# Attention in a fused kernel: the shared block as two 64-column couples, reciprocals widened and transposed, and three moves of order

## What is computed

```
scores = scale * matmul(q, k.T)                        # 4 batches x 8 heads, 576 x 64
thresh = max(scores, -1) - tau
scores = where(scores >= thresh, scores, -1e9)
attn   = exp(scores - max(scores)); attn /= sum(attn) + 1e-9
x      = matmul(attn, v)                               # -> 2304 x 512
h      = relu(x @ w_in);  x = (h * h) @ w_out          # 512 -> 2048 -> 512
e      = argmax(x @ w_gate)                            # 8 experts
out    = gate * sigmoid(x @ w_output_gate)[e] * ((x @ w1[e]) @ w2[e])
```

## Time and profile before

| | |
|---|---|
| median of 3 runs | 1035.98 us (1035.89 to 1037.17) |
| the profiled execution | 1037.33 us, of which span 1035.5 |
| TensorE busy | 1004.8 us, 97% of the span |
| VectorE, ScalarE, GpSimd busy | 617.7, 590.7, 414.1 us |
| granted TensorE clock, mean | 0.997 |
| attention | the first 333 us |

### The profile page before, as it was taken

One profiled execution on the slowest core, in us unless ns is written; L12 is line 12 of the kernel. 1 busy time (PEld: TensorE's weight loads), 2 busy tenths in 40 slices (PEclk: granted clock), 3 DMA queues, 4 the chain that ended last, 5 costly groups with the idle time before them and its releaser, 6 DMA issues.

```text
span 1035.5 us, 19649 instructions
## 1 busy us (share of the span) xinstructions
PE 1004.8 (97%) x6923; PEld 835.6 (81%) x6923; DVE 617.7 (60%) x1204; ACT 590.7 (57%) x922; POOL 414.1 (40%) x725
## 2 busy tenths in 40 slices
PE   7999999999998999999999999999999999999996
PEld 5877877877876788888888888889978888888884
DVE  5778787877876433422322242234788777777773
ACT  4777777777776332322322232223548888888883
POOL 4777777777776000000000000000007666666763
PEclk9999999999999999999999999999999999999998
DMA  4222232332210310021002001103579256451110
GB/s 114 76 63 63 75 70 53 72 84 53 70 40 22 93 51 21 1 52 31 1 21 55 7 1 42 40 1 83 183 269 396 105 203 240 153 194 41 33 41 34
DMA packets 85387, 84.07 MB, mean 81 GB/s; under 512 B 49711, under 2 KB 64559, under 8 KB 85298
## 3 DMA queue, kind: packets, MB, share of 16 engines
q1 hardware_dynamic: 81778, 72.41, 23.7%
q0 software_dynamic: 3520, 10.49, 3.0%
HBM read 69.24 MB, written 15.21 MB: 82 GB/s over the span
## 4 chain that ended last, share of the span: by engine, by line
PE 65%; DVE 1%; SPq 0%; issue 0%; DMA 0%; ACT 0%; POOL 0%; ACTq 0%; POOLq 0%
PE y_ps L1163 19%; PE h_ps L1146 19%; PE y_ps L1227 15%; PE row_ps L1227 7%; PE h_ps L1258 2%; PE row_ps L1132 2%; PE y_ps L1217 1%; DMA y_rows<-r_buf 0%; SPq L965 0%; SPq L961 0%; PE h_ps L1132 0%; POOL out_dram L1054 0%; DVE y_row L1697 0%; DVE g_lo L1484 0%; DVE g_buf L1479 0%
## 5 line engine op out<-in xcount | busy, mean ns | idle before, releaser
L1479 DVE TENSOR_TENSOR g_buf<-r_buf 128x512 f32<-128x512 f32 (+1 forms) x80 | 51.1, 639 | 222.0 <-ACT r_buf L1331 221.3
L1331 ACT ACTIVATE r_buf<-h_ps 128x512 f32<-128x512 f32 (+1 forms) x80 | 44.4, 555 | 235.3 <-PE h_ps L1146 231.8
L947 POOL TENSOR_TENSOR w_lo<-w_experts,w_hi 128x2048 fp32r<-128x2048 f32 x20 | 125.1, 6255 | 78.3 <-ACT w_hi L1390 78.2
L1390 ACT ACTIVATE w_hi<-w_experts 128x2048 fp32r (+1 forms) x100 | 150.4, 1564 | 0.5 <-PE row_ps L1227 0.5
L1065 POOL MEMSET ones<- 128x128 bf16 x1 | 0.2, 209 | 357.9 <-DVE x_lo L1465 357.9
L947 DVE TENSOR_TENSOR w_lo<-w_experts,w_hi 128x1024 fp32r<-128x1024 f32 (+1 forms) x80 | 136.9, 1753 | 4.5 <-ACT w_hi L1390 4.2
L476 ACT ACTIVATE e_sb<-s_sb,stats,live 128x576 f32<-128x576 f32 x144 | 124.5, 866 | 20.9 <-POOL stats L262 19.6
L1146 PE MATMUL h_ps<-x_hi,w_in_hi 128*128 128x512 f32 (+1 forms) x320 | 119.9, 375 | 2.3 <-DVE x_lo L1465 2.3
L1163 PE MATMUL y_ps<-g_hi,w_out_hi 128*128 128x512 f32 (+1 forms) x320 | 118.0, 369 | 1.6 <-DVE g_lo L1484 1.6
L1146 PE MATMUL h_ps<-x_hi,w_in_lo 128*128 128x512 f32 (+1 forms) x320 | 117.9, 369 | 0.0
L1146 PE MATMUL h_ps<-x_lo,w_in_hi 128*128 128x512 f32 (+1 forms) x320 | 117.8, 368 | 0.0
(11 more groups left out here) (250 smaller groups left out, 2226.1 us busy)
## 6 DMA issues: line engine op xcount, KB each, us to landing
w_experts<-in_moe_w_dram SPq DMA_DIRECT2D x18, 2048.0 KB, 9.6
y_rows<-y_row SPq DMA_DIRECT2D x36, 128.0 KB, 2.5
k_raw<-in_k_dram SPq DMA_DIRECT2D x32, 128.0 KB, 3.1
q_raw<-in_q_dram SPq DMA_DIRECT2D x32, 128.0 KB, 3.0
w_raw<-in_moe_w_in_dram SPq DMA_DIRECT2D x16, 256.0 KB, 3.1
v_nat<-in_v_dram SPq DMA_DIRECT2D x16, 256.0 KB, 2.7
y_T<-in_moe_w_out_dram SPq DMA_DIRECT2D x16, 256.0 KB, 2.8
y_early<-y_row SPq DMA_DIRECT2D x32, 128.0 KB, 2.4
```

What stands on the lines that cost most here:

```text
L947: alu.tensor_tensor(group_of(w_lo, g)[:, c0:c1], raw_group(buf, g)[:, c0:c1], group_of(w_hi, g)[:, c0:c1].bitcast(F32), ALU.subtract).then ...
L1390: nc.scalar.activation(group_of(w_hi, g)[:, c0:c1], raw_group(buf, g)[:, c0:c1], ACT.Copy).then_inc(hi_done, 1)
L1479: V.tensor_tensor(g_buf[:, 0:cols], r_buf[:, 0:cols], r_buf[:, 0:cols], ALU.mult).then_inc(sq_done, 1)
```

## The change

Five edits, all in attention.

1. The product with `v_mix` is made as two products of 64 columns, one for each half of the array, in place of one of 128.
2. `rinv` grows from nine numbers per partition to nine times 64. The reciprocal reads each sum 64 times and writes it 64 times.
3. `broadcast_rinv` makes four 128 x 128 transposes of `rinv` in place of eight 64-column products with the identity.
4. On TensorE `output_tail` stands ahead of the third transpose set of its step.
5. On VectorE the reciprocal stands ahead of `k_lo`; on GpSimd `add_eps` stands ahead of `cuts`.

```diff
-        rinv = sb("rinv", [P, CHUNKS])
+        rinv = sb("rinv", [P, CHUNKS, D])
...
                     biases(i, c)
-                    cuts(i, c)
                     if c == 0 and i >= 1:
                         add_eps(i - 1)
+                    cuts(i, c)
...
-                pe.matmul(o_ps[:, cols], v_mix[b][:], pt[:, LAST, :], start=False, stop=(c == LAST - 1),
-                          skip_group_check=True).then_inc(pv_done, 1)
+                for par in range(2):
+                    last = pe.matmul(o_ps[D * par:D * (par + 1), cols], v_mix[b][:, D * par:D * (par + 1)], pt[:, LAST, :],
+                                     start=False, stop=(c == LAST - 1), skip_group_check=True)
+                last.then_inc(pv_done, 1)
...
                 for c in range(LAST):
-                    for par in range(2):
-                        last = pe.matmul(m_ps[D * par:D * (par + 1), c * P:(c + 1) * P],
-                                         rinv[:, 2 * c + par:2 * c + par + 1].broadcast_to([P, D]), ident[:],
-                                         start=True, stop=True)
+                    last = pe.transpose(m_ps[:, c * P:(c + 1) * P],
+                                        rinv[:, 2 * c:2 * c + 2, :].rearrange("p h d -> p (h d)"), ident[:])
...
+                if 0 <= used[0] and used[1] == LAST:
+                    output_tail(used[0])
                 if 0 <= made[0] < PAIRS and sets_in(made[1]) == 3:
                     transposed_probs(*made, 2)
                 if c == 1 and i + 1 < PAIRS:
                     transposed_q(i + 1)
-                if 0 <= used[0] and used[1] == LAST:
-                    output_tail(used[0])
...
-                V.reciprocal(rinv[:], sums_eps[:]).then_inc(rinv_ready, 1)
+                V.reciprocal(rinv[:], sums_eps[:].rearrange("p (n a) -> p n a", a=1).broadcast_to([P, CHUNKS, D])
+                             ).then_inc(rinv_ready, 1)
...
+                if c == 0 and i >= 1:
+                    reciprocal(i - 1)
                 if c == 0 and i + 1 < PAIRS:
                     k_lo(i + 1)
-                if c == 0 and i >= 1:
-                    reciprocal(i - 1)
```

More of the change, by code:

```diff
@@ L416, in output_tail @@
                     pe.matmul(m_ps[D * par:D * (par + 1), TAIL:2 * TAIL],
-                              rinv[:, CHUNKS - 1:CHUNKS].broadcast_to([P, D]),
+                              rinv[:, CHUNKS - 1, :],
                               ident[:, par * TAIL:(par + 1) * TAIL], start=True, stop=True)
```

## The result

The changed kernel takes 1094.63 us, median of 4 runs (1093.94 to 1096.45), against 1036.07 before: 1.0566 times as long, 95% interval 1.0547 to 1.0584, or 58.6 us. The forecast was 1061, its range ended at 1088. The direction and the place were right, the size was not.

The account below looks back on a forecast made before the run. TensorE, busy 97% of the span, was taken as the bound. Fourteen pairs at +1.62 us (22.7), the fifteenth +0.7, the last +1.5 and the first mixes -0.2 made +24.7, so 1061 us; range 1046 to 1088.

Parts of the forecast that it names:

- TensorE slows after each hole: Rival: work behind each 2.8 us TensorE idle runs 1.56 times slower, +1.9 us in 14 pairs, 1088 us; chance 0.03.
- The reciprocal, the term that decides: VectorE's 576-element reciprocal takes 3.43 us; with k_lo behind it, TensorE's broadcast starts 2.59 us later in a pair.
- The cheap reciprocal: Rival: VectorE's wide reciprocal streams at 1.04 ns an element, 0.76 us, so the kernel gets faster, some 1020.5 us; chance 0.12.
- (a): TensorE's broadcast of rinv: four transposes in place of eight 64-column products save 0.58 us a pair.
- (b): TensorE's v_mix product as two 64-column couples saves 0.10 to 0.11 us a chunk, 0.32 a pair.
- (c): output_tail ahead of the third transpose set covers TensorE's wait for a bank's evacuation, saving 0.47 us a pair.
- (d): VectorE's masks of step 1 come later, so TensorE waits 0.40 us a pair for them before its second transpose set.
- VectorE as the bound: Rival: VectorE's 3.21 us of extra work a pair can't fill its idles, a pair grows by 2.26, 1072 us; chance 0.05.

Follow-up runs that it names:

- e_fill28: The changed kernel with 28 idle identity transposes into a free bank at the head of each broadcast; 1069.66 us (1.0328).
- e_probe: The kernel before with eight reciprocals, 9 to 576 elements wide, added to VectorE's setup; 1042.73 us, a single run.
- e_tail: The kernel before with one edit, the tail's products ahead of the third transpose set on TensorE; 1035.09 us (0.9988).

## Why the prediction was wrong, point by point

**The step that failed** is the rival "TensorE slows after each hole", which had 0.03 with the words "Against: busy share would stay about 85%". Busy share was no argument: it came out as said (18.63 of 21.90 us is 85%, in a pair that kept the clock), and the clock fell in twelve others all the same. The forecast had a 2.8 us idle piece in every pair, where no whole pair of before has one of over 0.6, and still took the lower level as out of reach. It came behind 12 of the 14 holes that ended with k_lo, behind the last two as well, and cost 25 us (`e_fill28`). This rival was the mechanism. Its price of 1.9 us a pair came from 3.4 us of slowed work, for which it named no row, and stood near the measured 1.3 to 2.5 of a pair that had it.

The rival's own evidence was better than the prediction took it for. In the kernel before, four transposes of k or q:

```profile
6.93 1.12 PE L312 MATMUL m_ps<-ident,k_raw 128*128 128x128 f32 x4 [3.36 <-DMA q_raw<-in_q_dram]
...
116.56 0.60 PE L322 MATMUL m_ps<-ident,q_raw 128*128 128x128 f32 x4
```

The 1.12 us behind the hole at the start is what four transposes take in the slowed pair above too (114.00). So TensorE ran at the pace of the lower level there although the granted clock shows 1.00, and that 1.00 was no evidence against the rival.

**The reciprocal, the term that decides.** Right in kind: an element costs about six plain ones, TensorE waits for reciprocal and k_lo in turn, 14 times for k_lo and twice for the reciprocal alone. Predicted 3.43 us, measured 3.75, since 5.67 ns an element is 6.25: 0.32 us sixteen times, 5 us. Start to release was to be 111.96 to 116.08, 4.12 us, and is 4.44, the same 0.32. The cheap reciprocal, which had 0.12 and would have made the change faster, is out by `e_probe`.

**Terms (a) and (b).** From the release to the q transposes 2.35 us with the clock kept, where it was 3.07 (113.49 to 116.56): -0.72, predicted -0.58 and -0.11. Term (b) was 0.05 a place and not 0.10, since the sum left out that the first instruction behind a change of shape pays 0.05. The broadcast gains the same 0.06, since the transposes behind it no longer pay it. With the q transposes paying it and two more places that count, (a) and (b) save 0.77 a pair, predicted 0.90.

**Terms (c) and (d).** The wait for the evacuation went: from the six transposes to the next scores it takes 2.27 us (185.58 to 187.85) where it took 2.66, -0.39, predicted -0.47. The wait for the masks came: in the pair that kept the clock, 0.33 us (188.85: a block of six takes 1.20, not 0.87), predicted 0.40. `e_tail` alone gains the predicted 0.07 a pair.

**The sum without the clock.** Predicted 1.62 a pair, measured 2.17 (21.90 less 19.73). Of the 0.55, 0.32 is the reciprocal's length and 0.08 its start (2.65 us behind the maximum's, where 109.39 to 111.96 is 2.57); (a) and (b) saved 0.13 less, (c) 0.08 less, and (d) cost 0.07 less. So 33.6 us in place of 24.7: some 1070, a little over the forecast's own 1069 and well inside the range; the clock's 25 made it 58.6.

**The moves of order** gave the reciprocal its earlier start (2.65 us behind the maximum's start; it was 3.83) and alone make the kernel 3.4 us faster.

**VectorE as the bound** didn't come: it idles 3.52 us before q_lo in a slowed pair, for ScalarE's q_hi, which waits for TensorE's q transposes.

## What to carry to other kernels

Before an instruction on a side engine is widened to save work on the bound one, read its price per element from two rows of different width, and look at what the bound engine does meanwhile. If the answer is "nothing, for microseconds, in each turn of the loop" in a kernel whose TensorE had no such pause, the lower clock belongs in the forecast and not among the remote rivals; products that nobody needs, into a free bank, show its share in one run. When a wait is covered by moving work into it, look for the next operand in line: here the masks took back six sevenths of the gain until one VectorE instruction was moved as well.

## What was not expected of the hardware

- Twelve of 14 idle pieces of 3.17 us on TensorE, in attention that was otherwise dense, were followed by stretches at half clock, and so were ten of 14 with 1.92 us left idle; with none, no pair of the loop was slowed.
- A float32 reciprocal on VectorE costs 6.25 ns an element from 72 elements on and 5.8 between 9 and 18; a source read with a stride of zero costs the same as a plain one. The copy of the same 576 numbers takes 0.75 us.
- Around a change between 64-column couples and 128 x 128 products the starts lie 0.2 us apart where 0.11 is usual, and the first instruction of the new shape takes 0.05 us longer.
- In the first 17 us of the kernel before, transposes run at half their usual pace (1.12 us for four, later 0.60) while the granted clock shows 1.00.
